# The order of the two bodies of a branch on two queues, in a linear-attention and double-MLP kernel

## What is computed

```python
for t in range(S):                                  # S = 768; state is 48 x 48 for each batch and head
    cur = einsum('bhd,bhe->bhde', u * k[t], v[t])
    y[t] = einsum('bhd,bhde->bhe', r[t], state + cur)
    state = w[..., None] * state + einsum('bhd,bhe->bhde', k[t], v[t])
x = y.transpose(0, 2, 1, 3).reshape(3072, 384)
x = ((x @ w_a) * (x @ w_b)) @ w_out                 # 384 -> 1536 -> 384
h = x @ w_in
out = (h * clip(h + 3, 0, 6) / 6) @ w_out2          # 384 -> 2048 -> 384
```

## Time and profile before

| | |
|---|---|
| median of 3 runs | 943.11 us (942.43 to 943.45) |
| the profiled execution, its own time | 942.92 us |
| its span, first to last instruction | 941.1 us |
| PE busy | 930.9 us (99%) |
| DVE, ACT, POOL busy | 369.4, 329.6, 179.5 us |
| granted TensorE clock | 0.999 of full speed |

### The profile page before, as it was taken

One profiled execution on the slowest core, in us unless ns is written; L12 is line 12 of the kernel. 1 busy time (PEld: TensorE's weight loads), 2 busy tenths in 40 slices (PEclk: granted clock), 3 DMA queues, 4 the chain that ended last, 5 costly groups with the idle time before them and its releaser, 6 DMA issues.

```text
span 941.1 us, 13441 instructions
## 1 busy us (share of the span) xinstructions
PE 930.9 (99%) x5568; PEld 764.2 (81%) x5568; DVE 369.4 (39%) x588; ACT 329.6 (35%) x652; POOL 179.5 (19%) x160
## 2 busy tenths in 40 slices
PE   9999999999999999999999999999999999999996
PEld 8788888888888888878888888888888888888885
DVE  7655434524442444333232334343343343343331
ACT  6544323232223233323221243343343333333332
POOL 4974201210211110100455590000000000000000
PEclk9999999999999999999999999999999999999999
DMA  8543103121112113013121120100200200100001
GB/s 290 189 141 118 51 34 101 52 84 52 52 51 85 51 51 102 34 51 118 59 76 46 64 93 1 34 34 0 68 1 1 68 1 20 48 1 1 34 0 37
DMA packets 24036, 56.33 MB, mean 60 GB/s; under 512 B 2336, under 2 KB 8224, under 8 KB 23968
## 3 DMA queue, kind: packets, MB, share of 16 engines
q1 hardware_dynamic: 19568, 46.74, 15.5%
q10 hardware_dynamic: 4400, 8.65, 2.4%
HBM read 45.95 MB, written 9.44 MB: 59 GB/s over the span
## 4 chain that ended last, share of the span: by engine, by line
PE 98%; DMA 1%; POOL 0%; DVE 0%; ACT 0%; issue 0%; POOLq 0%; DVEq 0%
PE up_ps L624 32%; PE up_ps L702 21%; PE acc_ps L638 16%; PE acc_ps L716 10%; PE att_ps L716 10%; PE att_ps L526 2%; PE att_ps L571 1%; PE att_ps L584 1%; PE att_ps L589 1%; PE att_ps L579 1%; PE up_ps L662 1%; DMA w_raw<-in_moe_w_a 1%; PE att_ps L557 1%; POOL prod L469 0%; DVE first_rk L927 0%; PE acc_ps L540 0%
## 5 line engine op out<-in xcount | busy, mean ns | idle before, releaser
L624 PE MATMUL up_ps<-x_cut,w_up 128*128 128x512 f32 x1296 | 310.1, 393 | 0.7 <-ACT x_cut L766 0.7
L624 PEld LDWEIGHTS up_ps<-x_cut,w_up 128*128 128x128 f32 x1296 | 240.7, 188 | 54.9 <-issue 3.0
L819 ACT ACTIVATE g_cut<-tmp 128x512 fp32r<-128x512 f32 x168 | 106.2, 632 | 219.8 <-DVE tmp L1027 147.1
L1035 DVE SCALAR_TENSOR_TENSOR g_cut<-tmp,g_cut 128x512 fp32r<-128x512 f32 x168 | 125.5, 747 | 117.3 <-ACT g_cut L819 117.3
L638 PE MATMUL acc_ps<-g_cut,w_down 128*128 128x512 f32 x648 | 158.2, 391 | 0.0
L638 PEld LDWEIGHTS acc_ps<-g_cut,w_down 128*128 128x128 f32 x648 | 120.8, 188 | 26.5 <-issue 1.0
L1029 DVE SCALAR_TENSOR_TENSOR tmp<-tmp,up_ps 128x512 f32<-128x512 f32 x96 | 66.1, 688 | 182.9 <-ACT tmp L813 182.9
L813 ACT ACTIVATE tmp<-up_ps,three 128x512 f32<-128x512 f32 x96 | 66.2, 690 | 171.1 <-PE up_ps L702 171.1
L1027 DVE TENSOR_TENSOR tmp<-tmp,up_ps 128x512 f32<-128x512 f32 x72 | 49.5, 688 | 184.4 <-PE up_ps L624 184.4
L702 PE MATMUL up_ps<-x_cut,w_up 128*128 128x512 f32 x432 | 105.7, 389 | 0.0
L702 PE MATMUL up_ps<-x_cut,w_in_first 128*128 128x512 f32 x432 | 105.4, 389 | 0.0
(11 more groups left out here) (110 smaller groups left out, 570.1 us busy)
## 6 DMA issues: line engine op xcount, KB each, us to landing
nat<-in_natural SPq DMA_DIRECT2D x20, 704.0 KB, 6.0
rkT<-in_rk_turned SPq DMA_DIRECT2D x20, 448.0 KB, 4.0
w_raw<-in_moe_w_out SPq DMA_DIRECT2D x28, 192.0 KB, 2.4
layer_out_T<-stage ACTq DMA_DIRECT2D x6, 768.0 KB, 3.4
x_cut<-layer_out_T SPq DMA_DIRECT2D x6, 768.0 KB, 4.3
outT<-stage ACTq DMA_DIRECT2D x5, 768.0 KB, 3.3
w_raw<-in_moe_w_in SPq DMA_DIRECT2D x12, 256.0 KB, 4.7
first_rk<-in_rk_turned SPq DMA_DIRECT2D x4, 448.0 KB, 5.8
```

Of the source, the lines that this page charges most:

```text
L624: mm = pe.matmul(up_ps[:, m, :], w_up[i // PB][:, a, m, c, cols], x_cut[:, t % 2, b, c, :], start=(z == 0), stop=(z == len(order) - 1))
L819: nc.scalar.activation(g_cut[:, n % GR, HI, :], tmp[:, n % 2, :], ACT.Copy, scale=1.0 if n < TILES * N1 else 1.0 / 6.0).then_inc(s_gh, 1)
L1035: dve.scalar_tensor_tensor(out=lo, in0=tmp[:, n % 2, :], scalar=1.0 if n < TILES * N1 else 1.0 / 6.0, in1=hi.bitcast(F32), op0=ALU.mult, o ...
```

## The change

On SP and on ACT the test of the flag is turned around and the two bodies change places. POOL, PE and DVE stay as they were.

```diff
                 flag_sp = decide(sp)
-                with sp.If(flag_sp == 1):
+                with sp.If(flag_sp == 0):
+                    sync_general(sp)
+                with sp.Else():
                     sync_fast(sp)
-                with sp.Else():
-                    sync_general(sp)
...
                 flag_act = decide(act)
-                with act.If(flag_act == 1):
+                with act.If(flag_act == 0):
+                    scalar_general(act)
+                with act.Else():
                     scalar_fast(act)
-                with act.Else():
-                    scalar_general(act)
```

## The result

The changed kernel takes **948.34 us** (median of 6 runs, 946.52 to 949.09) against 943.11 us before (6 runs, 942.43 to 943.96). The ratio is 1.0052, with a 95% interval of 1.0039 to 1.0065: slower, by 5.2 us. The profiled execution took 948.37 us with a span of 946.6. The forecast was 940.8 with a range of 939.9 to 943.1, so it missed in sign and in size.

The account below looks back on a forecast made before the run. PE, busy 99% of the span, was taken to bound the middle, leaving head and tail: -2.5 + 0 + 0 + 0.1 = -2.4 from 943.11 gives 940.7, plus 0.1 for a longer head jump: 940.8 us, range 939.9 to 943.1.

Parts of the forecast that it names:

- Tail of SP, removed: End of SP's program: without the jump the drain comes 2.5 us earlier; the branch left costs between nothing and POOL's 0.2.
- ACT's tail: End of ACT's program: its own jump gone, drain about 934.4 instead of 936.4, worth nothing, hidden under SP's wait.
- Head of SP, added: SP's start: jump of 2.6 us delays first loads to 8.1, hidden by 4.3 us of DMA backlog; cost 0.
- Head of ACT, added: ACT's start: jump of 2.7 us, 2.5 free in an existing wait, so 0.2 late; cost 0.
- Rival C: Head: fetch queues in the loads' line, jump 7.0 us, total +0.6 to +1.5, 943.7 to 944.6 us; chance 0.08.
- B: Head gives back 0.7 to 2.0 us through fetches on the late DMA engine or longer jumps, 941.4 to 942.7; chance 0.26.
- The cover: Head: 4.3 us of queueing behind first_loads would hide SP's late issues, as long as the jump takes under about 4 us.
- up to about 4.5 little does: ACT's head: with a jump up to 3.0 us nothing behind ACT moves, and up to about 4.5 little moves.
- Bandwidth, added: DMA in the head: two target blocks and probably two behind them, 8 KB each; cost 0.1 us, bounds 0 to 2.8.

Follow-up runs that it names:

- short_general: The changed kernel with the general bodies of SP and ACT cut to one wait, so the jump passes one instruction: 940.97 us, ratio 0.9975.
- SP alone: Kernel before with only SP's two bodies changing places, ACT as before: 949.53 us, ratio 1.0063.
- ACT alone: Kernel before with only ACT's two bodies changing places, SP as before: 949.6 us, ratio 1.0062.
- common_tail: Kernel before, its order of bodies kept, with SP's layer 2 issues standing once behind the If: 940.73 us, ratio 0.9968.
- after_quiet: The changed kernel with all loads but w_u, the first two first_rk and the masks moved behind the decision: 945.31 us, ratio 1.0016.
- act_late: Kernel before, no jump in the head, with ACT making nine spare copies first: 947.76 us, ratio 1.0050.
- after_warm_20: The changed kernel with 20 unread matmuls in PE's gap between the scores of chunk 1 and the outputs of chunk 0: 950.04 us, a single execution.
- after_warm: The changed kernel with 26 unread matmuls in PE's gap between the scores of chunk 1 and the outputs of chunk 0: 947.77 us, ratio 1.0046.
- sp_late_branch: Kernel before with only SP's bodies turned and all of SP's early issues moved ahead of its decision: 941.5 us, ratio 0.9979.
- after_warm_13b: Second profile of the changed kernel with 13 unread matmuls in PE's gap: 949.94 us, a single execution.
- before_again: Second profile of the unchanged kernel before, taken for the spread of its start: 946.67 us.
- sp_only_again: Second profile of the kernel before with only SP's two bodies changing places: 948.19 us, a single execution.
- after_warm_13: The changed kernel with 13 unread matmuls in PE's gap between the scores of chunk 1 and the outputs of chunk 0: 948.75 us, ratio 1.0046.

## Why the prediction was wrong

**Tail of SP, removed: right.** Taken were 2.5 us with bounds of 2.4 and 2.6; measured 2.4, and the two kernels that do this alone gain 2.1 and 2.8 us by their medians. The branch left behind the last body is executed, and the drain follows 0.2 behind it, POOL's value, the upper of the two bounds. ACT's tail was worth nothing, as argued.

**"Head of SP, added" and "Head of ACT, added": the steps that failed.** Both took the jump's price from the quiet tail, 2.6 and 2.7 us, and found it covered, "Cost 0". It was 6.7 to 6.8, of which 4.8 to 4.9 passed before the fetch was served, and the two steps together cost 7.9 to 8.1 us. The row that should have warned was already quoted: the loads of the same stretch took 6.7 us to land where a quiet one takes 2.4. Rival C, which put the fetch in that same line, gave 2.7 + 4.3 = 7.0 us for the jump, and was right within 0.3, as it was with the times at which the engines go on (12.4 and 12.1; measured 12.17 and 11.97). It was set at 0.08 on the strength of `first_k`, which shows what one block does to a load that is being served, not how long a block must wait.

The Trainium skill's rule on DMA queues, weighed under B (DMA: Bandwidth & Descriptors, "Queues, rings and completion order"), made a fetch wait one turn only. No turn was measured here; what was measured is a jump of 2.7 to 2.9 us at a DMA share of 0.12 and of 6.7 at 1.00, with 0.9 to 1.0 and 4.8 to 4.9 us before the packet is served, so whatever the turn is, it does not spare a fetch the wait behind the loads. The other rule (Runtime: NRT & Kernel Launch, "Instruction fetch mechanics"), that a taken branch to a block that isn't held fetches before it goes on, agrees with the long jumps here: each has a packet of the instruction queue before the engine goes on, and the short one of `short_general` has none there. It gives no price.

**The cover, and C's own sum: too small.** C forecast 3 to 3.9 us for the head; it was 7.9 to 8.1. It said too that the change is over 0.2% slower only with a jump of more than 7.3 us; with 6.8 it was 0.5% slower. C took the larger of the two delays. In truth they follow each other on one path, and the rows of the changed kernel give it. ACT 4.3 us late makes DVE's masks late, and DVE scales the r and k of chunks 2 and 3 at 17.89 instead of 14.02. DVE's timeline before:

```profile
14.02 2.33 DVE L927 TENSOR_TENSOR first_rk<-first_rk,tab_rk 112x1024 f32<-112x1024 f32 x2
```

in the changed kernel:

```profile
17.89 2.35 DVE L927 TENSOR_TENSOR first_rk<-first_rk,tab_rk 112x1024 f32<-112x1024 f32 x2
```

and POOL's:

```profile
20.31 2.78 POOL L242 TENSOR_TENSOR w_up<-w_raw,w_up 128x256 fp32r<-128x256 f32 x4 [6.89 <-DVE first_rk L927]
```

POOL cuts piece 0 at 20.31 and not 16.42, and SP issues piece 6 at 21.07 and not 17.18: 3.9 us. There the piece finds a line that is longer, since SP's own loads were 6.7 us late and the DMA stood partly idle before them (C's "dry for 3.0 us"): `nat` and `rkT` are issued at 18.29 and 19.91, right ahead of it, where they were 5 us ahead of it before. It takes 9.2 us in place of 6.7: 2.5 more. The prediction had counted on the line to hide a late issue; here it added to it. It reaches ACT at 30.3 instead of 23.9, 6.4 late. By the distances of before (0.64 us from the piece to `x_cut`, 0.52 from `x_cut` to L624) the weights alone would let layer 1 start at about 30.32 + 0.64 + 0.52 = 31.5, an estimate. The last 1.4 us up to 32.93 are PE's own: its chunks end late, after it was idle for 3.51 us and then ran at half clock. In the profile of `short_general`, where ACT and SP go on in time, 3.4 us at half clock (20.7 to 24.1) go with a layer 1 that starts 1.75 us late (26.79); what the 13.7 us here would cost by themselves no run shows. No case of the prediction had a term for the clock.

So "up to about 4.5 little does" was wrong in kind too. The prediction looked for the one to whom ACT's lateness passes, found DVE's mask with 0.5 us of slack, and then counted slack of ACT against its own waits; but behind those 0.5 us the path DVE, POOL, piece 6 has none, as the earlier trace rows shows, since it is the chain that ended last.

**"Bandwidth, added": the count right, the cost not measured.** From 5 to 13 us q14 brings four packets of 8 KB in the changed kernel (10.06, 10.33, 12.60 and 12.74 us) and none in the kernel before, which are the two targets and the two behind them. Over the whole run the count grows by one only, since the tail fetches less (23 packets where it was 22). No late landing of a neighbour stands out, but the 0.1 us can't be told apart from the rest.

**What stays open.** How the loss divides for SP alone: its three terms (dry DMA, late pieces, clock) were not seen in an ordinary start. Why SP alone costs 8.9 us at the head and both together 7.6, which is hardly beyond the intervals; ACT alone, with 6.6, does not cost more than both, it only lacks the tail's gain. Whether the fetch waits in one line with the loads or is held up by them in another way. And why TensorE starts slowly in some executions.

## What to carry to other kernels

A jump over a body that is longer than what the engine holds had the price of one small DMA in the traffic of that moment: 2.5 to 2.9 us where the queues were quiet, 5.5 to 6.8 behind a backlog. So put it where the engine has slack or the DMA is quiet, and let what both ways have in common stand once behind them (`common_tail`), in place of choosing which end of the program pays. When a wait is moved into a head full of loads, follow the chain that ended last through every engine and back into the DMA, and add the delays on it: lateness of an issue and length of the line it joins come one behind the other, and a gap on TensorE can cost again in clock.

## What the runs showed of the hardware

- A taken jump to instructions that aren't held: 2.5 (SP) to 2.9 us (DVE) in the quiet tail, 2.7 to 2.9 in a quiet head, 5.5 at 13.7 us and 6.6 to 6.8 at 5.1 to 5.4 us behind the first loads. It does not matter whether SP issues further loads behind the branch (ACT alone: 6.6).
- Such a jump has two parts: the wait until its packet of 8 KB is served (0.9 us in the tail, 0.9 and 1.0 in the quiet head, 3.7 at 13.7 us, 4.8 to 4.9 behind the first loads) and 1.6 to 1.9 us from there until the engine goes on.
- Behind a branch whose target is the next instruction SP drains 0.2 us later.
- TensorE behind an idle time of 3.51 us was granted half clock for some 13.7 us (16.0 to 29.7), and with one of 2.04 us (`after_quiet`, until 14.6) for as long (14.2 to 27.8); behind 2.25 us and one more of 0.47 (`act_late`) for 3.4 us (17.5 to 20.9); behind the start of one of 3.73 us (`after_warm_20`) for 6.8 (31.1 to 37.9). Behind 2.18 us (`after_warm`) and 1.52 us (`sp_late_branch`) it stayed at 1.00, and in `after_warm_13b` it fell from 9.8 to 13.3 us with no idle time over 0.22 us from 5 us on. So the length of the idle time alone doesn't tell what the clock will do.
- 13 and 20 float32 matmuls of 128 columns stand as 26 and 40 in the rows, 3.17 and 4.73 us, 0.12 each.
- In every profile here TensorE begins at about half speed, until 6 to 7 us in the ordinary ones. In `before_again`, `act_only`, `sp_only`, `sp_only_again` and `after_warm_13` this lasts until 15 to 21 us, with no idle time ahead; it costs the kernel before 3.6 us. The windows read 1.00 there for want of a record.
